# Moving the two large weight tables of a two-stage kernel to other byte addresses in SBUF

## The chip, the cores and the metric

One core of a Trainium2 chip runs the whole program. The metric is the device time of one execution in microseconds (us), the median over runs. The profile shown comes from one profiled execution of the same program.

## The reference, cut to what matters

```python
for t in range(S):                                   # first half: attention
    state = gamma * state + k[t] outer v[t]
    y[t] = scale * q[t] @ state
x = y as [3072 tokens, 512]
h = x @ w_in1                                        # [3072, 1024]
solu = h * softmax(h); ln = layernorm(solu) * g      # still first half
y = ln @ w_out1                                      # [3072, 512]
h2 = y @ w_in2                                       # second half: [3072, 2048]
out = (h2 * cos(h2)) @ w_out2                        # [3072, 512]
```

Batch is 4, heads 8, sequence 768, head size 64; everything is float32.

## The kernel before, in words

**Products.** Every operand of a product is kept as a high and a low part of about float32 together (`x_h`, `x_l`), and the helper `products` (lines 318, 320 and 321) issues three matmuls per term: high by high, high by low, low by high. The first factor is the stationary operand (128 x 128, loaded by a weight load), the second is the moving operand (384 or 512 columns in the large products). Three such matmuls are called a triple here. All of them read 4-byte elements.

**First half.** Tokens go in 24 tiles of 128. Per tile: the attention products (256 columns wide and 128 wide), then `h = x @ w_in1` as L1a and L1b (four triples each, moving `w1i_h`, `w1i_l`, stationary `x_h`, `x_l`), softmax and layernorm pieces on VectorE and ScalarE over the tile `work`, transposes by TensorE, and the second product L2a and L2b (eight triples in all, moving `w1o_h`, `w1o_l`, stationary `z_h`, `z_l`). The order over the engines is written out by hand in the list STEP. The result goes to a scratch in HBM by the DMA `y_scratch<-work` (L408). That makes 24 x (8 + 8) = 384 triples of 512 columns with weights of the first half as moving operand.

**Second half.** Tokens go in 4 superblocks of 768. A superblock has 8 passes j. A pass does 14 triples of 384 columns (a Strassen-like form: stationary `ring`, moving `yc_h`, `yc_l`; function `l3`), and between them, by the list FILL, 12 triples of 512 columns for the output product (function `l4`: stationary `glo_h`, `glo_l`, `ghi_h`, `ghi_l`, moving `w2o`). FILL puts the 12 in six groups of 1, 1, 3, 1, 3 and 3, each between ring triples. Each triple of `l4` adds to another PSUM bank than the triple before it; the triples of one L1a or L2a add to one bank. That makes 4 x 96 = 384 triples of 512 columns with `w2o` as moving operand. The last superblock ends with 18 `w2o` triples in a row. VectorE and ScalarE compute `h2 * cos(h2)` beside it.

**Memory.** The program has two overlapping layouts: tiles named by `sb1` for the first half and by `sb3` for the second, both laid one behind the other from byte 16512 of each partition, every tile starting at a multiple of 32 bytes. Tiles that are never read (`to_64_bytes`, `to_w1i`, `to_w2o`) only push what follows. In this kernel the start bytes of what matters are:

| tile | start byte | remainder by 512 |
|---|---|---|
| `q_h`, `k_h`, `v_h`, `p_h`, `s_h` and their low parts | 50304 and on | 128 |
| `w1i_h`, `x_h`, `work`, `z_h`, `w1o_h` and the like | 120544 and on | 224 |
| `ring`, `yc_h`, `yc_l` | 34944, 63616, 85120 | 128 |
| `c_32`, `gg`, `glo_h`, `ghi_h` and low parts | 119744 and on | 448 |
| `w2o` | 163328 | 0 |

All steps between operands inside these tiles (a block of 128 columns, a row of 384 or 512) are multiples of 512 bytes, so each tile's remainder is the same for every matmul that reads it.

**Transfers of the second half's output weights.** `w2o` is filled once, by eight DMAs of 1 MB on SP's queue (`load_w2o`, L496); the first goes out before the first half ends, the next two after the last store of `y`, the others in the first superblock.

```python
def load_w2o(j):
    sp.dma_start(w2o[:, slot_of(j):slot_of(j) + 2, :, :]..., w2o_split...[j, :, :, :])
...
m = products(pe, ps_out[:, t, :], [
    (h[:, cols], l[:, cols], w2o[:, slot_of(j) + r, 0, :],
     w2o[:, slot_of(j) + r, 1, :])],
    f == 0, f == NF - 1)
```

Of the kernel before, what the change touches and what calls it, by code (L numbers as in the profile page):

```python
# [94 lines left out]
def build(nc, qT, kT, kn, vn, consts, w1_in, w1_out, g_ln, w2_in, w2_out, y_scratch, w2_split,  # L95
          w2o_split, out):
    ctx = ExitStack()
    with ctx:
# [15 lines left out]
        with ExitStack() as one:  # L114
            def sb1(name, shape, dt=F32):
                return one.enter_context(nc.sbuf_tensor(name, shape, dt))


            w1_raw = sb1("w1_raw", [128, W1_SLOTS, 1024])
            sb1("behind_w1_raw", [128, 256])  # L120
            raw = sb1("raw", [128, 2, 4, 512])
            q_h = sb1("q_h", [128, 2, PAIRS, 2, C], F32R)
            q_l = sb1("q_l", [128, 2, PAIRS, 2, C], F32R)
            k_h, k_l = sb1("k_h", [128, 2, 512], F32R), sb1("k_l", [128, 2, 512], F32R)
            n_h, n_l = sb1("n_h", [128, 2, 512], F32R), sb1("n_l", [128, 2, 512], F32R)
            v_h, v_l = sb1("v_h", [128, 2, 512], F32R), sb1("v_l", [128, 2, 512], F32R)
            p_m = sb1("p_m", [128, 2, 512])
            p_h, p_l = sb1("p_h", [128, 2, 512], F32R), sb1("p_l", [128, 2, 512], F32R)
            s_32 = sb1("s_32", [128, 512])
            s_h, s_l = sb1("s_h", [128, 2, 512], F32R), sb1("s_l", [128, 2, 512], F32R)  # L130
            cst = sb1("cst", [128, NCONST])
            sb1("to_64_bytes", [128, 4])
            w1i_h = sb1("w1i_h", [128, KD, FF1], F32R)
            w1i_l = sb1("w1i_l", [128, KD, FF1], F32R)
            x_h, x_l = sb1("x_h", [128, 2, KD, C], F32R), sb1("x_l", [128, 2, KD, C], F32R)
            work = sb1("work", [128, 4, 1024])
            ident = sb1("ident", [128, 128])
            z_h, z_l = sb1("z_h", [128, K1, C], F32R), sb1("z_l", [128, K1, C], F32R)
            w1o_h = sb1("w1o_h", [128, K1, DM], F32R)
            w1o_l = sb1("w1o_l", [128, K1, DM], F32R)  # L140
            g_col = sb1("g_col", [128, K1])
            nmax, esum = sb1("nmax", [128, 2]), sb1("esum", [128, 2])
            esum1, rinv = sb1("esum1", [128, 2]), sb1("rinv", [128, 2])
            usum, nmu = sb1("usum", [128, 2]), sb1("nmu", [128, 2])
            ssq = sb1("ssq", [128, 2])
            scl = sb1("scl", [128, 2, 4])
            mhalf, warm = sb1("mhalf", [128, 1]), sb1("warm", [128, 1])
# [9 lines left out]
        with ExitStack() as three:  # L157
            def sb3(name, shape, dt=F32):
                return three.enter_context(nc.sbuf_tensor(name, shape, dt))


            y_raw = sb3("y_raw", [128, KD, SUPER])
            t_32 = sb3("t_32", [128, 2, 2, HALF])
            ring = sb3("ring", [128, 2, 7, 2, 2, 128], F32R)
            yc_h = sb3("yc_h", [128, 7, 2, HALF], F32R)
            yc_l = sb3("yc_l", [128, 7, 2, HALF], F32R)
            e_1, e_2 = sb3("e_1", [128, HALF]), sb3("e_2", [128, HALF])
            e_5 = sb3("e_5", [128, HALF])
            o_a = sb3("o_a", [128, 4, DM])
            sb3("to_w1i", [128, 80])  # L170

            c_32 = sb3("c_32", [128, 2, 2, HALF])
            turns = sb3("turns", [128, 2, SUPER], I32)
            gg = sb3("gg", [128, 2, SUPER])
            glo_h, glo_l = sb3("glo_h", [128, SUPER], F32R), sb3("glo_l", [128, SUPER], F32R)
            ghi_h, ghi_l = sb3("ghi_h", [128, 2, SUPER], F32R), sb3("ghi_l", [128, 2, SUPER], F32R)
            o_b = sb3("o_b", [128, 2, DM])
            sb3("to_w2o", [128, 656])

            w2o = sb3("w2o", [128, NF, 2, DM], F32R)  # L180

# [1219 lines left out]
```

How the kernel before makes its waits and increments, by code:

```python
        def wait(eng, s, batch, tile, per=1, i=0, per_batch=TILES):  # L285
            value = batch * (per_batch * per) + (tile * per + i + 1)
            if not isinstance(value, int):
                assert value.min_val >= 1
                eng.wait_ge(s, value)
            elif value > 0:
                eng.wait_ge(s, value)
# [43 lines left out]
        def loaded(eng, loads, t, b):  # L337
            eng.wait_ge(loads[t % 2], b * (32 * TILES // 2) + 32 * (t // 2 + 1))
# [47 lines left out]
            def load_w1(u):  # L387
                if u >= W1_SLOTS:
                    sp.wait_ge(w1_lo, u - W1_SLOTS + 1)
                dst = w1_raw[:, u % W1_SLOTS, :]
                if u < KD:
                    sp.dma_start(dst, w1_in[u * 128:(u + 1) * 128, :]).then_inc(ld_w1[u], 16)
                else:
                    k = 2 * (u - KD)
                    src = w1_out[k * 128:(k + 2) * 128, :].rearrange("(k p) n -> p k n", k=2)
                    sp.dma_start(dst.rearrange("p (k n) -> p k n", k=2), src)\
                        .then_inc(ld_w1[u], 16)
# [1 line left out]
            def load_next(t, par):  # L399
                sp.wait_ge(n_lo, t + 1)
                sp.wait_ge(q_lo[1], t + 1)
                load_tile(t + 2, par)
# [1 line left out]
            def store_yt(t):  # L405
                src = yt_of.get(t, yt32) if isinstance(t, int) else yt32
                sp.wait_ge(ytc_done, t + 1)
                sp.dma_start(y_scratch.rearrange("(k p) t -> p k t", k=KD)[
                    :, :, bass.ds(t * C, C)], src.rearrange("p (k t) -> p k t", k=KD))\
```

## Time and profile before

| | |
|---|---|
| median of 3 runs | 958.75 us (958.66 to 959.32) |
| profiled execution, its own time | 958.3 us |
| its span, first to last instruction | 956.5 us |
| mean granted TensorE clock | 0.993 of full speed |
| TensorE matmul busy | 931.4 us, 97% of the span, 4992 matmuls |
| VectorE busy | 732.5 us, 77% |
| ScalarE busy | 563.0 us, 59% |

A matmul's busy time starts when its operands begin to stream and ends when its last result is written, so consecutive matmuls overlap in the record; the distance between two starts is what a matmul costs. TensorE's weight loads (PEld) run beside the matmuls.

### The profile page before, as it was taken

To read this page: it belongs to the slowest core of one execution; us is meant where nothing else is said; L and a number is where in the kernel's file an instruction comes from. 1 tells how busy PE (TensorE), PEld (TensorE's weight loads), DVE (VectorE), ACT (ScalarE), POOL (GpSimd) and SP (SyncE) were. 2 spreads that over 40 slices of the span, in tenths; PEclk is the share of its full clock that TensorE was granted. 3 is DMA by queue.
4 is the path that set the end of the run, shared out by engine and by line. 5 is a ranking of instruction groups with operands and counts; after the bars stand their busy time and mean duration, and the time that the engine had idled before them with its cause. 6 is when DMAs were issued, how large, how long until landed. Compare 5 with 4: busy or idle time off the path is not lost.

```text
span 956.5 us, 14711 instructions
## 1 busy us (share of the span) xinstructions
PE 931.4 (97%) x4992; PEld 826.1 (86%) x4992; DVE 732.5 (77%) x1054; ACT 563.0 (59%) x923; POOL 265.3 (28%) x260
## 2 busy tenths in 40 slices
PE   4799999999999999999999999999999999999998
PEld 3688888888888888888989898889889898989897
DVE  8989899999999899987656586566766566766564
ACT  5656657657657567546645475555665455656453
POOL 2365576666675666742000000000000000000000
PEclk8899999999999999999999999999999999999999
DMA  7423453633653554528786344734446444454301
GB/s 278 154 66 116 140 214 138 199 131 137 209 202 115 173 178 156 183 84 275 245 310 215 111 122 130 234 111 125 114 123 220 145 117 121 114 182 121 110 11 66
DMA packets 106520, 148.18 MB, mean 155 GB/s; under 512 B 7408, under 2 KB 77040, under 8 KB 106480
## 3 DMA queue, kind: packets, MB, share of 16 engines
q1 hardware_dynamic: 106480, 147.69, 47.5%
q8 instruction: 20, 0.33, 0.1%
q14 instruction: 20, 0.16, 0.1%
HBM read 112.01 MB, written 35.65 MB: 154 GB/s over the span
## 4 chain that ended last, share of the span: by engine, by line
PE 81%; DVE 12%; issue 4%; ACT 1%; DMA 1%; POOL 0%; DVEq 0%; SPq 0%; ACTq 0%; POOLq 0%
PE bank L318 26%; PE bank L321 26%; PE bank L320 26%; DVE p_l L1111 2%; DVE q_l L1095 1%; PE bank L620 1%; DVE work L1161 1%; DVE p_m L1104 1%; DVE x_l L1135 1%; DVE nmax L1155 1%; DVE wo_out L1209 1%; PE bank L655 1%; DVE z_l L1189 1%; ACT x_h L788 1%; DVE work L1201 1%
## 5 line engine op out<-in xcount | busy, mean ns | idle before, releaser
L321 PE MATMUL bank<-yc_h,ring 128*128 128x384 f32 x448 | 150.6, 336 | 0.0
L320 PE MATMUL bank<-yc_l,ring 128*128 128x384 f32 x448 | 150.5, 336 | 0.0
L318 PE MATMUL bank<-yc_h,ring 128*128 128x384 f32 x448 | 150.3, 336 | 0.0
L1238 DVE SCALAR_TENSOR_TENSOR gg<-turns,c 128x768 f32<-128x768 int32 x64 | 61.1, 954 | 63.8 <-ACT turns L859 63.8
L1035 POOL TENSOR_TENSOR y_raw<-y_raw,t 128x768 f32<-128x768 f32 x4 | 7.4, 1851 | 362.0 <-DVE yc_l L1220 362.0
L865 ACT ACTIVATE gg<-gg 128x768 f32<-128x768 f32 x64 | 54.2, 847 | 81.0 <-DVE gg L1245 80.9
L859 ACT ACTIVATE turns<-c 128x768 int32<-128x768 f32 x64 | 54.2, 847 | 80.5 <-DVE c L1308 78.0
L318 PEld LDWEIGHTS bank<-yc_h,ring 128*128 128x128 f32 x448 | 84.2, 188 | 8.3 <-issue 0.4
L320 PEld LDWEIGHTS bank<-yc_l,ring 128*128 128x128 f32 x448 | 84.1, 188 | 8.1
L321 PEld LDWEIGHTS bank<-yc_h,ring 128*128 128x128 f32 x448 | 84.1, 188 | 0.0
L318 PE MATMUL bank<-w1i_h,x_h 128*128 128x512 f32 x192 | 78.5, 409 | 5.0 <-DVE x_l L1135 3.6
L318 PE MATMUL bank<-w1o_h,z_h 128*128 128x512 f32 x192 | 77.3, 403 | 0.0
L321 PE MATMUL bank<-w1i_h,x_l 128*128 128x512 f32 x192 | 76.2, 397 | 0.0
L318 PE MATMUL bank<-w2o,ghi_h 128*128 128x512 f32 x192 | 76.1, 396 | 0.0
L318 PE MATMUL bank<-w2o,glo_h 128*128 128x512 f32 x192 | 75.9, 395 | 0.0
L320 PE MATMUL bank<-w1i_l,x_h 128*128 128x512 f32 x192 | 75.7, 394 | 0.0
L321 PE MATMUL bank<-w1o_h,z_l 128*128 128x512 f32 x192 | 75.6, 394 | 0.0
L320 PE MATMUL bank<-w2o,ghi_h 128*128 128x512 f32 x192 | 75.6, 394 | 0.0
L321 PE MATMUL bank<-w2o,ghi_l 128*128 128x512 f32 x192 | 75.5, 393 | 0.0
L321 PE MATMUL bank<-w2o,glo_l 128*128 128x512 f32 x192 | 75.4, 393 | 0.0
L320 PE MATMUL bank<-w2o,glo_h 128*128 128x512 f32 x192 | 75.1, 391 | 0.0
L320 PE MATMUL bank<-w1o_l,z_h 128*128 128x512 f32 x192 | 75.0, 391 | 0.0
(131 smaller groups left out, 2487.1 us busy)
## 6 DMA issues: line engine op xcount, KB each, us to landing
ring<-w_split SPq DMA_DIRECT2D x224, 256.0 KB, 2.8
w_split<-w_out SPq DMA_DIRECT2D x16, 896.0 KB, 4.7
w2o_split<-wo_out SPq DMA_DIRECT2D x16, 512.0 KB, 4.1
w2o<-w2o_split SPq DMA_DIRECT2D x8, 1024.0 KB, 8.0
raw<-kT SPq DMA_DIRECT2D x24, 256.0 KB, 2.7
raw<-qT SPq DMA_DIRECT2D x24, 256.0 KB, 3.0
raw<-kn SPq DMA_DIRECT2D x24, 256.0 KB, 3.9
raw<-vn SPq DMA_DIRECT2D x24, 256.0 KB, 4.3
```

Of the source, the lines that this page charges most:

```text
L318: eng.matmul(dst, ah, bh, start=first and i == 0, stop=False, skip_group_check=read_between)
L320: eng.matmul(dst, ah, bl, start=False, stop=False, skip_group_check=read_between)
L321: m = eng.matmul(dst, al, bh, start=False, stop=last_one and i == n - 1, skip_group_check=read_between)
L620: m = pe.transpose(ps_t[:, k * 128:(k + 1) * 128], c_b[:, (4 * g + k) * 128:(4 * g + k + 1) * 128], ident[:, :])
L655: m = pe.transpose(ps_t[:, k * 128:(k + 1) * 128], y32[:, k * 128:(k + 1) * 128], ident[:, :])
L788: m = act.copy(x_h[r, par, 2 * g:2 * g + 2, :], two_pairs(ps_o[r, :])[:, :, a, :])
L859: act.activation(turns[:, r, :], flat(c_32[:, r, :, :]), ACT.Copy, scale=INV_2PI)\
L865: act.activation(gg[:, r, :], gg[:, r, :], ACT.Sin, scale=0.5)\
L1095: dve.tensor_tensor(q_l[64:128, par, :, 1, :], raw[64:128, par, 0, :].rearrange("p (c t) -> p c t", c=PAIRS), q_h[64:128, par, :, 1, :].bi ...
L1104: dve.tensor_tensor(two_pairs(p_m[:, g, :]), two_pairs(ps_p[:, g, :]), mask[:, 4 * g:4 * g + 4, :].rearrange("p (j a) t -> p j a t", j=2), ...
L1111: dve.tensor_tensor(p_l[:, g, :], p_m[:, g, :], p_h[:, g, :].bitcast(F32), ALU.subtract).then_inc(pl_done, 1)
L1238: dve.scalar_tensor_tensor(gg[:, r, :], turns[:, r, :], -TWO_PI_HI, flat(c_32[:, r, :, :]), ALU.mult, ALU.add)\
```

## The change

Two filler tiles get other sizes. In the first layout everything behind `cst` starts 352 - 32 = 320 bytes later (the filler of 4 floats takes 32 bytes with the rounding, that of 84 floats 352). In the second layout `w2o` starts 144 floats, 576 bytes, earlier. No instruction, wait, shape or order changes.

```diff
             cst = sb1("cst", [128, NCONST])
-            sb1("to_64_bytes", [128, 4])
+            sb1("to_512_bytes", [128, 84])
             w1i_h = sb1("w1i_h", [128, KD, FF1], F32R)
             w1i_l = sb1("w1i_l", [128, KD, FF1], F32R)
             x_h, x_l = sb1("x_h", [128, 2, KD, C], F32R), sb1("x_l", [128, 2, KD, C], F32R)
...
             o_b = sb3("o_b", [128, 2, DM])
-            sb3("to_w2o", [128, 656])
+            sb3("to_w2o", [128, 512])

             w2o = sb3("w2o", [128, NF, 2, DM], F32R)
```

New start bytes: `w1i_h` 120864 and what follows it, remainder 32 by 512; `w2o` 162752, remainder 448. The other rows of the table above keep theirs.

## Rows read from the trace of the kernel before

**Rows 1.** The page: busy time, share of the span, instructions.

```profile
PE 931.4 (97%) x4992; PEld 826.1 (86%) x4992; DVE 732.5 (77%) x1054; ACT 563.0 (59%) x923; POOL 265.3 (28%) x260
```

**Rows 2.** Stretches: busy us (count) of PE, PEld, DVE, ACT, POOL; clock, DMA, GB/s.

```profile
100.00:240.00 140.00, 138.28 (x814) 120.59 (x813) 129.53 (x201) 89.19 (x163) 90.86 (x92) 1.00 0.47 159
565.00:690.20 125.20, 125.20 (x625) 112.52 (x624) 81.87 (x102) 71.54 (x107) 1.85 (x1) 1.00 0.48 143
```

**Rows 3.** Timeline: first matmul of superblocks 2, 3 and 4 (start us, us).

```profile
564.93 0.33 PE L318 MATMUL bank<-yc_h,ring 128*128 128x384 f32 x1
...
690.22 0.33 PE L318 MATMUL bank<-yc_h,ring 128*128 128x384 f32 x1
...
815.49 0.33 PE L318 MATMUL bank<-yc_h,ring 128*128 128x384 f32 x1
```

**Rows 4.** The ring's tile, one superblock: duration ns min/median/max, first and last start.

```profile
L318 PE MATMUL bank<-yc_h,ring x112: 332/334/337, 564.9 to 687.6; 128*128 128x384 f32 x112
```

**Rows 5.** The tile w2o in the same superblock.

```profile
L320 PE MATMUL bank<-w2o,ghi_h x48: 388/397/397, 567.3 to 683.5; 128*128 128x512 f32 x48
L321 PE MATMUL bank<-w2o,ghi_l x48: 392/394/394, 567.5 to 683.7; 128*128 128x512 f32 x48
L318 PE MATMUL bank<-w2o,glo_h x48: 394/394/398, 575.4 to 689.5; 128*128 128x512 f32 x48
```

**Rows 6.** The tile w2o in the last run of 54 matmuls.

```profile
L318 PE MATMUL bank<-w2o,glo_h x6: 394/394/394, 944.9 to 948.3; 128*128 128x512 f32 x6
L320 PE MATMUL bank<-w2o,glo_h x6: 388/388/388, 945.1 to 948.6; 128*128 128x512 f32 x6
L321 PE MATMUL bank<-w2o,glo_l x7: 392/392/392, 940.5 to 948.8; 128*128 128x512 f32 x7
```

**Rows 7.** Timeline of that run: two matmuls, 21 apart.

```profile
947.64 0.39 PE L318 MATMUL bank<-w2o,glo_h 128*128 128x512 f32 x1
...
952.45 0.39 PE L318 MATMUL bank<-w2o,ghi_h 128*128 128x512 f32 x1
```

**Rows 8.** Tiles w1o_h and w1o_l, first half, 140 to 240 us.

```profile
L318 PE MATMUL bank<-w1o_h,z_h x48: 389/396/478, 141.5 to 236.5; 128*128 128x512 f32 x48
...
L320 PE MATMUL bank<-w1o_l,z_h x48: 387/389/395, 141.7 to 236.7; 128*128 128x512 f32 x48
```

**Rows 9.** Timeline: one triple of w1o late in an L2, then the next.

```profile
144.26 0.39 PE L318 MATMUL bank<-w1o_h,z_h 128*128 128x512 f32 x1
...
144.94 0.39 PE L318 MATMUL bank<-w1o_h,z_h 128*128 128x512 f32 x1
```

**Rows 10.** Timeline: w1o right behind ring matmuls, where the halves overlap.

```profile
450.52 0.34 PE L321 MATMUL bank<-yc_h,ring 128*128 128x384 f32 x1
450.70 0.40 PE L318 MATMUL bank<-w1o_h,z_h 128*128 128x512 f32 x1
...
451.17 0.40 PE L321 MATMUL bank<-w1o_h,z_l 128*128 128x512 f32 x1
451.40 0.39 PE L318 MATMUL bank<-w1o_h,z_h 128*128 128x512 f32 x1
```

**Rows 11.** Groups by line, VectorE: results at remainders 128 and 224.

```profile
L1189 DVE TENSOR_TENSOR z_l<-bank,z_h 128x512 fp32r<-128x512 f32 x48 | 32.6, 680 | 9.6 <-ACT z_h L812 9.5
...
L1104 DVE TENSOR_TENSOR p_m<-bank,cst 128x512 f32<-128x512 f32 x48 | 31.3, 686 | 4.5 <-PE bank L321 4.2
```

**Rows 12.** The tile w2o: its DMA issues, and their time to landing.

```profile
L496 SPq DMA_DIRECT2D w2o<-w2o_split x8: 379/471/1180, 440.2 to 516.5; - x8
...
DMA to landing us min/median/max: 5.0/8.0/10.1
```

**Rows 13.** Timeline of SP's queue: the loads of passes 1 and 2.

```profile
464.49 0.89 SPq L496 DMA_DIRECT2D w2o<-w2o_split  x2
```

**Rows 14.** Timeline of PE: first use of pass 0's weights, and of pass 1's.

```profile
463.62 0.40 PE L318 MATMUL bank<-w2o,glo_h 128*128 128x512 f32 x1
...
481.44 0.40 PE L318 MATMUL bank<-w2o,glo_h 128*128 128x512 f32 x1
```

## The prediction

> **What bounds the kernel now.** I read the page first, then busy time by stretch, then single tiles, because a change of addresses alone can act only through how long an instruction or a transfer takes. The page says that TensorE is busy 97% of the span [rows 1]. By stretch it is busy 138.28 of 140 us in the first half and without a gap through a superblock, at the full granted clock [rows 2]. The reader is to see that VectorE, the next busiest, has 43 us free in each superblock, so TensorE's own pace is the time there: a nanosecond on a matmul goes straight to the end, and one on another engine mostly does not. The pace is regular: superblocks 2, 3 and 4 begin 125.29 and 125.27 us apart [rows 3], the same to the resolution of the rows. Chance has no part in it, and a small shift by address would show as a clean step.
>
> **The change part by part.** It removes no instruction and adds none. It can act in four places: moving operands of matmuls, stationary operands, other engines on moved tiles, DMAs.
>
> *Moving operands at the remainders seen.* The distance between starts is what a matmul costs. A triple of `w1o` deep in an L2 takes 144.94 - 144.26 = 0.68 us [rows 9], 227 ns a matmul, durations down to 389 ns [rows 8]. In the last run of `w2o` seven triples take 952.45 - 947.64 = 4.81 us [rows 7], 0.687 us a triple or 229 ns a matmul, with durations 394, 388 and 392 [rows 6]. Against three times 389 ns that is 1174 - 1167 = 7 ns per triple, and 3 x 229 - 680 gives 7 as well. So `w2o` is a little slower than the first half's weights, in a run long enough to settle.
>
> What differs? In every other large product the stationary and the moving operand have the same remainder by 512 bytes (128 and 128 for the ring, 224 and 224 for L1 and L2). For `w2o` alone it is 0 against 448, and the change makes it 448 and 448. But `w2o` also is the only one that changes its PSUM bank after each triple. The trace does not separate the two. Bounds: if the remainder is the cause, 384 triples x 7 ns = 2.7 us are gained. If what is lost behind ring matmuls had the same cause, more: there the medians are 397 and 394 [rows 5], with 398 as the first one's maximum, so about 397 + 397 + 394 = 1188 against 1167, 21 ns, on 6 x 8 x 4 = 192 triples (FILL's groups), and 7 ns on the other 192: 4.0 + 1.3 = 5.4 us. Against the second: `w1o` behind the ring, its operands at equal remainders, shows the same durations of 0.40 us, two matmuls taking 451.17 - 450.70 = 0.47 us, where two settled ones take 0.45, and only the fourth is back at 0.39 [rows 10]. It recovers no sooner than `w2o`. So this part of the loss belongs to the passage from 384 to 512 columns, and equal remainders do not save it. Most `w2o` triples stand in groups of 1 to 3, so settled ones at equal remainders may never come about there; then only the last run gains, 18 x 7 = 126 ns. I take 0.1 us gain, and keep 0 and 5.4 as the ends.
>
> The Trainium skill says that TensorE has two independent read ports into SBUF, one for the moving operand and one for weight loads (SBUF — State Buffer, Who interferes with whom). By that rule the two streams of a triple cannot hinder each other at any pair of remainders, and the gain is 0 instead of up to 5.4 us. The trace neither proves nor refutes it: the 7 ns stand in the rows, their cause does not.
>
> *First half's weights.* `w1i`, `w1o` and their stationary partners `x` and `z` move together, from remainder 224 to 32, so equal stays equal. What may matter is the remainder itself. The trace has two values at equal pairs: 128 for the ring, whose durations lie within 332 to 337 ns [rows 4], and 224, that settles at 389 [rows 8]. Neither shows a cost of its own: both settle, and neither varies by more than a few nanoseconds. I take 0 from these two, the nearest rows. As an upper end I take the unsettled price of `w2o`, 7 ns on each of the 384 triples, 2.7 us slower, since in this half too TensorE is busy 99% [rows 2]; the far end, 21 ns on each, is 8.1 us. A lower end on this side is that passages into these products get cheaper: the first matmul's median is 396 against 389 at the least [rows 8], and 7 ns on each of 4 x 24 = 96 groups (L1a, L1b, L2a, L2b) are 0.7 us gained. Shifts are 320 and 576 bytes, both multiples of 64, so nothing that depends on a line of 64 bytes or less changes.
>
> *Other engines.* VectorE takes 686 ns for 512 columns into `p_m` (remainder 128) and 680 ns into `z_l` (224) [rows 11]. The few nanoseconds are those of different operands, so the moved `work`, `x`, `z` cost nothing more; were it 10 ns on each, the free time of VectorE in [rows 2] covers it for the second half, and in the first its work is 93% of the stretch beside TensorE's 99%, so a part would show, some tenths of a us over the 24 tiles.
>
> *DMAs.* The loads of `w2o` land within 5.0 to 10.1 us [rows 12]. Those of passes 1 and 2 go out from 464.49 to 465.38 [rows 13], so they land by 475.5 at the latest; pass 0's weights are used from 463.62 on and pass 1's, after all twelve triples of pass 0, from 481.44 [rows 14]: 6 us of cover, filled by TensorE's work on pass 0. The transfer would have to slow by more than half to be felt; with no cover, the whole of its lateness would stall TensorE once, not in each superblock, for the table is loaded once. I take 0. By the Trainium skill a transfer that does not start at a multiple of 256 bytes takes one extra partial transaction (DMA: Bandwidth & Descriptors, How a descriptor splits into AXI transactions); for 4096 bytes starting 192 past such a multiple that is an estimate of 134 beats for 128, 5% of a load, inside the cover.
>
> *Sum.* Profiled execution 958.3 (span 956.5 and 1.8 around it), minus 0.1, plus 0, plus 0: 958.2 us. The median of the runs lies 0.45 us above the profiled time, so 958.7 us by the runs. A difference under 0.2%, 1.9 us, is about what a measurement of this kernel cannot tell from no change.
>
> **The rivals.**
> *Equal remainders help (faster).* The stationary and the moving stream of `w2o` hinder each other at 0 against 448. For it: `w2o` is the only pair of unequal remainders and the only one that never settles at 389. Against it: the bank change per triple explains that too; [rows 10]. Price 2.7 us if the 7 ns go everywhere, 5.4 us if the passages go too: 956.0 to 953.3 us. It decides above 5 ns per triple (1.9 us over 384).
>
> *A start just behind a multiple of 512 is bad (slower).* `w2o` starts at remainder 0 and never settles; the first half's weights go to remainder 32, nearer to it than 224. If closeness to that boundary is what costs, the first half takes over the 7 ns while `w2o` at 448, 64 bytes short of it, keeps or loses them. With them kept: 384 x 7 ns = 2.7 us, 961.4 us. For it: nothing but the single value 0. Against it: the boundary is crossed by every operand of 512 bytes or more anyway, at 128 as at 224. It decides from 5 ns per triple of the first half; at 21 ns it would be 8.1 us, 966.8.
>
> *The filler does not do what its name says (no change).* `to_512_bytes` brings `w1i_h` to remainder 32, not 0. Whatever exact alignment might give the first half, it isn't reached. This ends where the forecast ends and strengthens it.
>
> **How the numbers follow.** No measurable change 0.53 (of which the filler's case is part), with its own range 956.8 to 960.6. Faster by over 1.9 us 0.27: it has a real irregularity of `w2o` on its side and two bounds, 2.7 and 5.4. Slower 0.20: the same size, with one value behind it, and all costs of an untried remainder. The time of the likeliest is 958.7. The range reaches to the faster rival's end, 953.3, and up past the slower rival's 961.4 to 962.5; about 2 in 10 remain outside, for passages dearer or cheaper than any row shows.
>
> **What would show it.** Right: superblocks again 125.3 us apart, `w2o` 394, 388, 392 in the last run, `w1o` and `w1i` settling at 389. Faster rival: `w2o` at 389 three times in the last run, superblocks at least 0.6 us shorter. Slower rival: no 389 in the first half, superblocks unchanged, the first superblock beginning later. Wrong in another way: an idle gap of TensorE at 481 us (a late load), or VectorE's durations on `work` changed. The forecast fails if the passages between ring and `w2o`, 48 in a superblock each way, depend on remainders in a manner that no row before can show.

## The result and the profile after

The changed kernel takes 956.17 us (median of 8 runs, 955.71 to 957.12), the kernel before 958.75 (958.57 to 959.51). The ratio is 0.9972 with a 95% interval of 0.9961 to 0.9983: 2.6 us, 0.28% faster, just beyond the 1.9 us called measurable. This is the first rival's case, not the likeliest of the forecast. The span of the profiled execution went from 956.5 to 954.4 us.

Stretches of the changed kernel, in the columns of [rows 2]:

```profile
100.00:240.00 140.00, 138.13 (x814) 120.34 (x813) 129.40 (x201) 88.70 (x162) 91.14 (x92) 1.00 0.46 160
565.00:689.50 124.50, 124.50 (x625) 113.11 (x624) 81.78 (x102) 71.44 (x107) 1.86 (x1) 1.00 0.49 144
```

TensorE is as full as before. In the first half the same number of matmuls, 814, falls into the stretch; in the second half the superblock itself is shorter. The timeline gives the first matmul of superblocks 2, 3 and 4:

```profile
564.96 0.34 PE L318 MATMUL bank<-yc_h,ring 128*128 128x384 f32 x1
...
689.54 0.34 PE L318 MATMUL bank<-yc_h,ring 128*128 128x384 f32 x1
...
814.13 0.34 PE L318 MATMUL bank<-yc_h,ring 128*128 128x384 f32 x1
```

Superblock 2 begins at 564.96 against 564.93 [rows 3]. That hides a gain: in this execution the last matmul of the first half starts at 460.69 us, before at 460.15 (among the kernels below whose first half is untouched it lies anywhere from 459.59 to 461.64), and from there to superblock 2 it is 104.27 us against 104.79. From then on the distance is 124.58 and 124.59 us, 0.69 us less each time, and the last superblock gains 0.81. Which matmuls gave it? The tile views, in the last run of `w2o`, then of `w2o` and of the ring through superblock 2:

```profile
L318 PE MATMUL bank<-w2o,glo_h x7: 389/389/389, 938.0 to 946.2; 128*128 128x512 f32 x7
L320 PE MATMUL bank<-w2o,glo_h x7: 389/389/389, 938.3 to 946.4; 128*128 128x512 f32 x7
L321 PE MATMUL bank<-w2o,glo_l x8: 389/389/393, 937.8 to 946.7; 128*128 128x512 f32 x8
...
L320 PE MATMUL bank<-w2o,ghi_h x48: 389/389/393, 567.3 to 682.9; 128*128 128x512 f32 x48
...
L320 PE MATMUL bank<-yc_l,ring x112: 333/334/346, 565.1 to 687.1; 128*128 128x384 f32 x112
```

The settled triple went from 394, 388, 392 ns [rows 6] to 389 three times, as the rival said. The median of the second matmul of a `ghi` triple went from 397 ns [rows 5] to 389: behind the ring, too, most of the loss is gone, which I had not expected. By the distances between starts in superblock 2, the first `w2o` triple of a group cost 703.5 ns before and 683.0 after, the other triples 687.5 and 681.5. And the ring, untouched, reaches 346 ns, where 337 ended its first line in [rows 4] and no line of it passed 340. From the distances between starts, each matmul to the next, over the 96 `w2o` triples and 112 ring triples of a superblock: `w2o` 695.4 ns per triple before and 682.3 after, ring 522.5 before and 527.6 after. That is -1.26 and +0.57 us, together -0.69. The ring's loss lies not in its first triple behind `w2o` (523.3 and 521.9 ns) but in those after it (521.8 and 531.8). Taken for all four superblocks, `w2o` gained 5.0 us over its 384 triples and the ring gave back 2.3 us over its 448.

The loads of `w2o` are as before and TensorE waits for none of them:

```profile
DMA to landing us min/median/max: 5.1/8.7/10.3
```

### The profile page after: what moved, and what is told of

The parts are those of the page before. It is cut to its first block, busy times and chain, and to the rows that moved or that the text cites. A ratio compares the mean times of both kernels' runs of the same rounds, so it can differ in the third digit from the quotient of the medians.

```text
span 954.4 us, 14711 instructions
## 1 busy us (share of the span) xinstructions
PE 929.9 (97%) x4992; PEld 828.8 (87%) x4992; DVE 732.1 (77%) x1054; ACT 562.7 (59%) x923; POOL 265.2 (28%) x260
## 4 chain that ended last, share of the span: by engine, by line
PE 79%; DVE 13%; issue 4%; ACT 2%; DMA 1%; POOL 0%; DVEq 0%; SPq 0%; ACTq 0%; POOLq 0%
PE bank L318 26%; PE bank L321 26%; PE bank L320 26%; DVE p_l L1111 2%; DVE q_l L1095 1%; PE bank L620 1%; DVE work L1161 1%; DVE p_m L1104 1%; DVE nmax L1155 1%; DVE x_l L1135 1%; DVE wo_out L1209 1%; PE bank L655 1%; ACT x_h L788 1%; DVE z_l L1189 1%; DVE s_l L1128 1%
## 5 line engine op out<-in xcount | busy, mean ns | idle before, releaser
L320 PE MATMUL bank<-w2o,ghi_h 128*128 128x512 f32 x192 | 74.9, 390 | 0.0
L318 PE MATMUL bank<-w2o,ghi_h 128*128 128x512 f32 x192 | 74.6, 388 | 0.0
```

The costliest lines, as they stand in the source:

```text
L318: eng.matmul(dst, ah, bh, start=first and i == 0, stop=False, skip_group_check=read_between)
L320: eng.matmul(dst, ah, bl, start=False, stop=False, skip_group_check=read_between)
```

## The experiments

All but the two tables are the kernel before with other filler sizes, some with one more filler. In each, the distances between the starts of TensorE's 624 matmuls repeat from superblock 2 to 3 within 2 ns, and the superblocks themselves within 1 ns, so the distance between superblocks is the sharpest measure, and the median says whether the rest agrees.

**Each move alone.**

```diff
-            sb3("to_w2o", [128, 656])
+            sb3("to_w2o", [128, 512])
```

> Only w2o moves, from remainder 0 to 448 by 512 (equal to its stationary partners glo and ghi); the first half's weights stay at 224. Theory 'equal remainders' and theory 'a moving operand that starts at remainder 0 is bad' both expect the whole gain here: superblocks 124.59 us apart as in the changed kernel, before 125.28, last run of w2o at 389, 389, 389 ns, median near 956.1 us. Theory 'the first half's weights bring the gain': no change, 958.7 us, superblocks 125.28.

956.16 us, ratio 0.9974 (0.9965 to 0.9984). The timeline's superblocks 3 and 4:

```profile
689.50 0.34 PE L318 MATMUL bank<-yc_h,ring 128*128 128x384 f32 x1
...
814.08 0.34 PE L318 MATMUL bank<-yc_h,ring 128*128 128x384 f32 x1
```

```diff
-            sb1("to_64_bytes", [128, 4])
+            sb1("to_64_bytes", [128, 84])
```

> Only the first layout moves, remainder 224 to 32; w2o stays at 0. If w2o brings the gain: superblocks 125.28 us apart, w2o 394, 388, 392, first half within 0.3 us of before, median 958.7 us within 0.2%. If remainder 32 costs the first half something (the slower rival): 960 to 961.4 us. If it brings the gain: 956.1 us.

958.78 us, ratio 1.0000 (0.9991 to 1.0009):

```profile
690.83 0.33 PE L318 MATMUL bank<-yc_h,ring 128*128 128x384 f32 x1
...
816.11 0.33 PE L318 MATMUL bank<-yc_h,ring 128*128 128x384 f32 x1
```

124.58 us with `w2o` moved, 125.28 with the first layout moved. The whole gain is `w2o`'s; the first half's move does nothing that the median can tell, and the slower rival falls.

**Equal remainders, or a bad start at 0?** First the partners come to `w2o` instead:

```diff
-            sb3("to_w1i", [128, 80])
+            sb3("to_w1i", [128, 96])
...
-            sb3("to_w2o", [128, 656])
+            sb3("to_w2o", [128, 640])
```

> The second half's gate tiles (c_32 to o_b) start 64 bytes later, so glo and ghi have remainder 0 as w2o has; nothing else moves. 'Equal remainders' expects w2o to settle at 389 ns three times in the last run and superblocks 0.5 to 0.8 us shorter than 125.28. 'A start at remainder 0 is bad' expects 394, 388, 392 still, and 125.28 us.

958.44 us, ratio 0.9995 (0.9986 to 1.0005). The last run of `w2o` settles at 389, with a distance of 226.7 ns. So a start at 0 is not what keeps `w2o` from settling. But the superblocks are 125.22 us apart, 0.06 less and not 0.5 to 0.8. `w2o` costs 688.3 ns per triple, 7.1 less than before, and the ring 528.2, 5.7 more: what `w2o` gained, the ring lost. The ring's own starts are unchanged, so it lost in the passages, the first matmuls behind a change between ring and `w2o`.

```diff
-            sb3("to_w2o", [128, 656])
+            sb3("to_w2o", [128, 576])
```

> w2o at remainder 192, stationary partners at 448: unequal, by 256, and not at 0. 'Equal remainders' expects w2o not to settle at 389 (as before, or another repeating pattern), superblocks 125.0 us or more. 'Remainder 0 is bad' expects 389 three times and about 124.6 us.

956.29 us, ratio 0.9974 (0.9964 to 0.9983), superblocks 124.59 us apart, each of the 624 distances between starts, averaged over superblocks 2 and 3, within 1 ns of the changed kernel's. Remainders 192 and 448 by 512 are unequal, so "equal by 512" is false. They are equal by 256. The other possibility, by 128, needs another distance:

```diff
-            sb3("to_w2o", [128, 656])
+            sb3("to_w2o", [128, 544])
```

> w2o at remainder 64 by 512, partners at 448: the distance is 128. If what counts repeats every 128 bytes: settles at 389 ns three times, superblocks 124.59 us, the pattern of the changed kernel. If it repeats every 256 bytes (which 448 and 192 cannot tell from 128): another pattern, not settled at 389 or a period other than 124.59.

959.24 us, ratio 1.0008 (0.9998 to 1.0017), superblocks 125.44 us. The last run, by tile:

```profile
L320 PE MATMUL bank<-w2o,ghi_h x6: 390/394/404, 949.9 to 953.3; 128*128 128x512 f32 x6
```

A distance of 128 doesn't settle at 389. What counts repeats every 256 bytes, as far as these starts tell.

```diff
-            sb3("to_w2o", [128, 656])
+            sb3("to_w2o", [128, 520])
```

> w2o at remainder 480, partners at 448: the distance is 32. 'Equal remainders by 128 settle, all else does not' expects an unsettled last run (a sum over 1167 ns per triple) and superblocks over 124.59 us. 'Only a distance of 64 is bad' expects 389 three times and about 124.6 us.

962.36 us, ratio 1.0038 (1.0026 to 1.0051), superblocks 126.24 us, matmuls of 393 to 397 ns to the end:

```profile
L320 PE MATMUL bank<-w2o,ghi_h x6: 393/395/397, 946.8 to 954.5; 128*128 128x512 f32 x6
```

A distance of 32 is worse than the 64 of before. So 64 was no special flaw; 0 is special.

**What do the passages cost?**

```diff
-            sb3("to_w1i", [128, 80])
+            pass
...
-            sb3("to_w2o", [128, 656])
+            sb3("to_w2o", [128, 640])
```

> All large operands of the second half at remainder 128: ring and yc as they are, glo and ghi from 448 to 128, w2o from 0 to 128. If only the remainder by 128 counts this is the same case as both at 0: superblocks 125.22 us, 389 three times in the last run. If a step in remainder by 512 between ring and w2o is what the passages cost: both passages fall towards nothing and superblocks come near 123.5 us (112 ring triples x 0.520 plus 96 x 0.680).

961.45 us, ratio 1.0029 (1.0018 to 1.0041), superblocks 126.08 us. The last run settles at 389. With no step in remainder between the large operands of the second half, the superblock is still longer than in any kernel above except the one with 480, and 2.6 us longer than settled triples alone would make it (112 x 0.520 + 96 x 0.680 = 123.5 us). So my second theory, that a step between the tiles is what the passages cost, is wrong.

```diff
+            sb3("to_yc", [128, 16])
             yc_h = sb3("yc_h", [128, 7, 2, HALF], F32R)
...
-            sb3("to_w1i", [128, 80])
+            sb3("to_w1i", [128, 64])
```

> Only yc_h and yc_l move, by 64 bytes, so the ring's triples have 128 against 192, a distance of 64, as w2o's had; w2o stays unequal too. If a distance of 64 between the stationary and the moving operand is what costs, ring triples inside their runs take some ns more than 520 ns (7 if it is as for w2o: 112 x 7 = 0.8 us per superblock, 126.1 us); if the loss is peculiar to 512 columns or to w2o: 125.28 us unchanged, within 0.1.

One run, 955.32 us; superblocks 124.48 us apart. A distance of 64 in the ring makes it cheaper, not dearer: 519.3 ns per ring triple against 522.5. And the `w2o` triples, whose own starts didn't move, fell from 695.4 to 690.9 ns, so more than half of the gain is in them. What holds for 512 columns does not hold for 384. (The tiles between `yc_l` and the filler, which VectorE and ScalarE use, moved by 64 bytes as well; the second table below, without them, gives the same 124.48.) Added to the change's own move of `w2o`:

```diff
-            sb3("to_w2o", [128, 656])
+            sb3("to_w2o", [128, 512])
```

> yc at remainder 192 (as in the run with yc alone) and w2o at 448 (as in the changed kernel). If the two gains are independent: superblocks 125.28 - 0.69 - 0.80 = 123.8 us, median near 953 us. If each run's pattern depends on what the passage before it left, they do not add: between 124.0 and 125.0 us. 'A distance of 64 is always bad' expects more than 124.59 us, against the run with yc alone.

957.25 us, ratio 0.9986 (0.9977 to 0.9995), superblocks 124.96 us. Two moves that gain 0.80 and 0.69 us alone gain 0.32 us together. They don't add: what a passage costs depends on the starts on both of its sides.

**TensorE by itself.** Two kernels hold nothing of the computation but matmuls on tiles that differ only in their start. The first runs 8 triples for each pair of starts:

```python
for n in (512, 384):
    for s in range(8):          # stationary at 32 * s
        for m in range(8):      # moving at 32 * m
            for i in range(8):
                triple(bank[:, i, 0:n], *operands(s, m, n), True)
```

> Leaves the whole computation out: only long runs of float32r triples, stationary and moving operand at each of 8 x 8 remainders by 256 in steps of 32, 8 triples each at 512 and at 384 columns, to alternating banks, then six pairs in one bank. 'Equal remainders by 256 settle': on the diagonal 227 ns a matmul (512 columns) and 173 (384), off it more where the weight load meets the moving operand; stationary 192 with moving 0 gives 229 (232, 226, 229), in one bank too. 'The bank change costs': 227 in one bank for every pair and 229 with alternating banks. 'w2o in particular': 227 everywhere.

Each cost is the distance between starts over 12 matmuls, from the 10th to the 22nd of a pair's 24. The timeline rows for stationary 192, moving 0 (the pair of the kernel before), and for 0 and 0:

```profile
303.22 0.39 PE L53 MATMUL bank<-mv_a,st_g 128*128 128x512 f32 x1
...
305.96 0.39 PE L53 MATMUL bank<-mv_a,st_g 128*128 128x512 f32 x1
...
35.71 0.39 PE L53 MATMUL bank<-mv_a,st_a 128*128 128x512 f32 x1
...
38.43 0.39 PE L53 MATMUL bank<-mv_a,st_a 128*128 128x512 f32 x1
```

2.74 against 2.72 us for 12. In nanoseconds of the trace that is 228.9 and 226.7 each. Over the 64 pairs the cost goes, with two exceptions, by the distance alone, moving minus stationary start by 256:

| distance in bytes | 0 | 32 | 64 | 96 | 128 | 160 | 192 | 224 |
|---|---|---|---|---|---|---|---|---|
| 512 columns, ns a matmul | 226.7 | 233.3 | 228.9 | 233.3 | 233.3 | 234.6 | 233.3 | 233.3 |
| 384 columns, ns a matmul | 173.3 | 173.3 | 173.3 | 176.7 | 175.8 | 176.7 | 174.5 | 173.3 |

All eight pairs of a distance agree within 0.5 ns, but for two at 384 columns: stationary 160 and moving 64 (distance 160) has 173.3, stationary 224 and moving 0 (distance 32) has 176.7. Why these two differ stays open. At distances of 128 and 160 the matmuls keep alternating (229 and 238 ns, for one), and another choice of 12 shifts the mean by up to 0.9 ns. In one bank the pair of before costs 228.9 too, with the same 232, 226, 229: the bank change that I held against the rival has no part in it.

The second kernel runs the matmuls of a pass in the order of FILL, with the ring at 128, for 70 sets of starts:

```python
CASES = [(4, y, g, g) for g in range(8) for y in range(8)]   # starts / 32: ring, yc, gates, weights
CASES += [(4, 4, 6, 0), (4, 4, 6, 2), (4, 4, 6, 7), (4, 6, 6, 0), (4, 4, 0, 0), (4, 4, 6, 6)]
```

> Leaves the whole computation out: TensorE's order of one pass of the second half (14 triples of 384 columns, 12 of 512 in groups of 1, 1, 3, 1, 3, 3) twice for each of 70 cases; ring at remainder 128, yc at 8 remainders, gate and output weights together at 8, then six mixed pairs. If addresses alone set the time, with no part for the other engines or DMAs, the six known cases give an eighth of their superblock: before 15.66 us, changed 15.57, output weights at 64 15.68, at 480 15.78, yc at 192 15.56, both at 0 15.65. If other engines take part, the cases come out alike or in another order.

A pass is the distance between the first 512-column matmul in its first run and the same one in its second. For the starts of the kernel before, of the changed one, and of the cheapest set:

```profile
2060.99 0.40 PE L62 MATMUL bank<-mv_a,st_g 128*128 128x512 f32 x1
...
2076.65 0.40 PE L62 MATMUL bank<-mv_a,st_g 128*128 128x512 f32 x1
...
2217.64 0.39 PE L62 MATMUL bank<-mv_g,st_g 128*128 128x512 f32 x1
...
2233.22 0.39 PE L62 MATMUL bank<-mv_g,st_g 128*128 128x512 f32 x1
...
1998.58 0.39 PE L62 MATMUL bank<-mv_h,st_h 128*128 128x512 f32 x1
...
2014.06 0.39 PE L62 MATMUL bank<-mv_h,st_h 128*128 128x512 f32 x1
```

15.66, 15.57 (in the trace's nanoseconds 15,573) and 15.48 us. Eight times each, beside what the full kernels showed:

| starts by 256: yc, gates, weights | 8 x pass | superblock in the full kernel |
|---|---|---|
| 128, 192, 0 (before) | 125.28 | 125.28 |
| 128, 192, 192 (changed) | 124.58 | 124.59 |
| 128, 192, 64 | 125.44 | 125.44 |
| 128, 192, 224 | 126.24 | 126.24 |
| 192, 192, 0 | 124.48 | 124.48 |
| 192, 192, 192 | 124.96 | 124.96 |
| 128, 0, 0 | 125.22 | 125.22 |
| 128, 128, 128 | 126.08 | 126.08 |

TensorE with nothing beside it gives all eight to 0.01 us. Where gates and weights have one start, the 64 sets lie between 15.48 and 15.76 us a pass, and I found no simple rule in the starts that orders them. Two sets share 15.48: yc at 192 with gates and weights at 224, and yc at 96 with them at 128. (In some of the 64 the two runs of the pass are not yet alike, and its length shifts by up to 0.1 us with the matmul taken; for the sets named here it is the same within 1 ns from the first 512-column matmul on.)

**A cheapest set in the full kernel.** Of the two, the one with 192 and 224:

```diff
+            sb3("to_yc", [128, 16])
             yc_h = sb3("yc_h", [128, 7, 2, HALF], F32R)
...
-            sb3("to_w1i", [128, 80])
+            sb3("to_w1i", [128, 72])
...
-            sb3("to_w2o", [128, 656])
+            sb3("to_w2o", [128, 512])
```

> The cheapest case of the passage table with the ring at 128: yc at remainder 192, glo, ghi and w2o at 224 by 256 (480 by 512). If the table of TensorE alone holds in the full kernel: 8 x 15.48 = 123.84 us per superblock, 1.44 below before and 0.75 below the changed kernel; the median near 958.8 - 4 x 1.44 = 953.0 us, faster than both. If the other engines or the semaphore waits take part: nearer 124.6 us and 956 us.

953.43 us (952.74 to 953.69), ratio 0.9941 (0.9928 to 0.9955), about twice the gain of the change:

```profile
688.57 0.33 PE L319 MATMUL bank<-yc_h,ring 128*128 128x384 f32 x1
...
812.41 0.33 PE L319 MATMUL bank<-yc_h,ring 128*128 128x384 f32 x1
```

123.84 us, as the table said.

## Why the prediction was right or wrong

**The bound** was right. Address effects of a few nanoseconds on a matmul arrived undiminished: 4 superblocks x 0.69 us = 2.8 us, against 2.6 between the medians. The spans of the two single profiles differ by 2.1 only because the changed kernel's execution reached the end of its first half 0.54 us later; behind it the trace shows 0.52 + 0.69 + 0.69 + 0.81 = 2.7 us.

**Range and sign.** 956.17 us lies within 953.3 to 962.5. It lies outside the likeliest case's own 956.8 to 960.6; that case, with 0.53, did not come true, and the faster rival, with 0.27, did. Its lower price of 2.7 us (956.0) matches what was measured, but by luck: it was 384 x 7 ns of settled loss, and the runs show -5.0 us on `w2o` and +2.3 us on the ring. Its upper price, 4.0 + 1.3 = 5.4 us for `w2o` with the passages, was nearly right for `w2o`: 192 triples x 20.5 ns and 192 x 6.0 ns make about 5. What the sum had no term for, in any of its cases, is what the move of `w2o` does to the ring, whose own starts stay.

**The step that failed** is the choice of 0.1 us for `w2o`, with its sentence that the loss behind the ring "belongs to the passage" and that equal remainders do not save it. Measured, 20.5 of the 23.5 ns that the first triple of a group lost are gone, and `w2o` gained 5.0 us. The sentence was read from one passage of `w1o` behind the ring [rows 10]: 0.40 us for each of three matmuls at equal remainders. The passage table shows why that row could not carry it. `w1o` stood at 224, and with the ring and yc at 128 a pair at 224 makes a pass of 15.760 us, as dear as any of the eight, while the pair at 192, where the change puts `w2o`, makes it 15.573. A pair of starts that the trace doesn't have was bounded by a row of another pair. The prediction did name this as the way in which it could fail: passages that depend on remainders in a manner that no row before can show.

**The bank change**, held against the rival, was wrong: alone in one bank the pair costs the same 228.9 ns.

**The ports.** The forecast set beside the trace a rule of the Trainium skill (SBUF — State Buffer, Who interferes with whom): the port of the moving operand and that of the weight loads are independent. The steady table disagrees with what I made of it: at 512 columns a matmul costs 226.7 or up to 234.6 ns by nothing but the distance between its two operands. The rule may still be true of the ports; the inference "so the pair of addresses cannot matter" is not.

**The first half** was right at 0: the ratio with its move alone is 1.0000. Stationary and moving operands kept their distance of 0, which the steady table makes 226.7 ns at every start. But the passages of the first half did change, and the zero is partly two shifts that cancel. The median of the first matmul of a `w1o` triple fell from the 396 ns of [rows 8] to 389, while that of `w1i_h` with `x_h` rose from 389 to 393:

```profile
L318 PE MATMUL bank<-w1o_h,z_h x48: 387/389/474, 141.9 to 237.0; 128*128 128x512 f32 x48
```

Between the 301st matmul and the first on the ring, the 486 on `w1o` took 113.69 us before and 113.20 after, start to start, and the 504 on `w1i` 119.36 and 119.88; with the first layout moved alone it is 113.17 and 119.83. Five of the kernels that leave the first half alone stay within 113.62 to 113.69 us on `w1o`. So of the gain of 0.7 us that the prediction kept as an end, 0.5 came about on `w1o`, and `w1i` took it back. With one sign for both, the half would have moved by 1 us.

**Other engines and DMAs** were right at 0. VectorE's 686 and 680 ns [rows 11] came out the same, the loads took at most 10.3 us, and from 465 us on TensorE waited for nothing. That the bare matmuls give every superblock to 0.01 us settles it for the second half: neither engines nor transfers take part.

**The fillers.** That `to_512_bytes` misses a multiple of 512 had no consequence, as nothing tested goes by 512.

**Still open** is what in TensorE or in SBUF repeats every 256 bytes, and whether it is the weight load or the stream that waits: every matmul here has its own weight load, and no run took one away. Open too is the rule of the passages: that the starts alone make them is shown by the second table, but they were tabulated, not explained.

## What to carry to other kernels

Where TensorE is full, look at the distance between starts of the same matmul in several places; if a settled run costs more than its neighbours of the same shape, compare the start addresses of its two operands by 256 bytes and make them equal for long runs. (This was seen with float32r operands and a weight load before every matmul; nothing else was tried.) For short groups of alternating shapes that rule isn't enough: equal starts ranged over 1.8% of a pass here, so try the sets of starts in a kernel that holds TensorE's matmuls alone, and take the cheapest to the full kernel. And look beyond the products whose operands move: here the ring, which didn't, took back nearly half of the gain. A filler tile is a free knob, but each tile behind it moves too, so a tuned layout is lost with any change of sizes ahead of it.

## What the runs showed of the hardware that was not expected

- The cost of a float32r matmul in a settled run depends on the distance between the starts of its moving and its stationary operand by 256 bytes: 226.7 ns at 0, 228.9 at 64, 233.3 to 234.6 at the others tried for 512 columns; 173.3 to 176.7 ns for 384 columns, where 0, 32, 64 and 224 cost the same but for one pair.
- After a change of width the matmuls settle only over several more (behind the ring, `w2o` at the starts before took 237, 235 and 231 ns before the settled round of 232, 226 and 229; in the changed kernel the ring took 172, 171, 175, 178, 185, 175 and 182 ns at the head of a run of twelve before it came to 173 and 174), and the loss or gain depends on the starts on both sides: one pass of 78 matmuls ran from 15.48 to 15.78 us. In superblocks 2 and 3 of all the full kernels single ring matmuls took 168 to 186 ns from start to start, and with the cheapest set a ring triple took 517.9 ns on average, so a passage can also fall below the settled 520.
- TensorE's timing repeats to a nanosecond or two: eight layouts timed in the full kernel and in bare matmuls agree to 0.01 us in 125.
